# Counting masks in a routing search on TensorE: three token blocks as one 120-column stationary part, totals by one matmul over ones, and the expert's first product issued earlier

## The reference

```python
# 1: linear attention with decay, B=4, H=8, S=768, head 48
for t in range(S):
    y[:, :, t] = einsum('bhd,bhde->bhe', rt, state + u * kt * vt)
    state = w * state + kt * vt
# 2: mixture of experts, N=3072 tokens, D=384, E=8, F=1024, cap = N // E = 384
for idx in argsort(-(x @ w_gate).flatten()):       # best (token, expert) pairs first
    tok, e = idx // E, idx % E
    if assigned[tok] >= 0 or counts[e] >= cap: continue
    assigned[tok] = e; counts[e] += 1
for e in range(E):
    out[assigned == e] = relu(x[assigned == e] @ w1[e]) @ w2[e]
# 3: bilinear layer, width 1536
return ((out @ w_a) * (out @ w_b)) @ w_out
```

## Time and profile before

| | us |
|---|---|
| median of 3 runs | 968.44 (968.01 to 969.39) |
| the profiled execution | 963.17 |
| its span, first to last instruction | 961.4 |
| TensorE busy in it | 899.6 (94%) |
| VectorE, GpSimd, ScalarE busy | 517.8, 474.4, 219.2 |

### The profile page before, as it was taken

One profiled execution on the slowest core, in us unless ns is written; L12 is line 12 of the kernel. 1 busy time (PEld: TensorE's weight loads), 2 busy tenths in 40 slices (PEclk: granted clock), 3 DMA queues, 4 the chain that ended last, 5 costly groups with the idle time before them and its releaser, 6 DMA issues.

```text
span 961.4 us, 17913 instructions
## 1 busy us (share of the span) xinstructions
PE 899.6 (94%) x6581; PEld 864.7 (90%) x6581; DVE 517.8 (54%) x1238; ACT 219.2 (23%) x454; POOL 474.4 (49%) x491
## 2 busy tenths in 40 slices
PE   5999999626999999999999999999999999999995
PEld 5999999515999999999999999899999999999995
DVE  7777777575656555555545565556455622442221
ACT  0212120002123221322222223122312322222221
POOL 5988897126316731781277037604750673277001
PEclk9999999856999999999999999999999999999998
DMA  5785754003001200210021012101210221022000
GB/s 104 210 220 117 197 122 107 19 33 107 18 19 65 66 33 33 74 49 25 33 82 57 8 45 86 49 0 55 76 49 0 72 73 36 34 83 66 1 1 25
DMA packets 92782, 61.19 MB, mean 64 GB/s; under 512 B 78800, under 2 KB 83536, under 8 KB 92752
## 3 DMA queue, kind: packets, MB, share of 16 engines
q0 software_dynamic: 11008, 34.61, 11.4%
q1 hardware_dynamic: 77872, 21.45, 9.7%
q10 hardware_dynamic: 3872, 4.72, 1.4%
HBM read 51.33 MB, written 9.44 MB: 63 GB/s over the span
## 4 chain that ended last, share of the span: by engine, by line
PE 74%; issue 9%; DVE 7%; POOL 5%; DMA 3%; ACT 2%; POOLq 0%; DVEq 0%; ACTq 0%
PE bank L1060 28%; PE bank L1103 11%; PE bank L1134 9%; PE bank L972 5%; PE bank L990 4%; PE bank L1017 3%; DMA wst<-in_moe_w,rows_i 3%; PE bank L948 2%; POOL w L478 2%; POOL wst L461 2%; PE bank L996 2%; PE bank L1116 2%; PE bank L982 2%; PE bank L962 2%; DVE ga L805 1%
## 5 line engine op out<-in xcount | busy, mean ns | idle before, releaser
L1060 PE MATMUL bank<-act,w_all 128*128 128x384 f32 x1584 | 295.5, 337 | 0.0
L1060 PEld LDWEIGHTS bank<-act,w_all 128*128 128x128 f32 x1584 | 275.0, 188 | 0.5
L461 POOL DMA_INDIRECT wst<-in_moe_w,rows_i x48 | 52.1, 1086 | 272.9 <-DVE rows_i L681 216.8
L1134 PE MATMUL bank<-w_all,gs 128*128 128x384 f32 x864 | 168.2, 339 | 0.6 <-DVE gs L808 0.5
L1134 PEld LDWEIGHTS bank<-w_all,gs 128*128 128x128 f32 x864 | 149.4, 188 | 2.0 <-DVE gs L808 1.5
L478 POOL TENSOR_TENSOR w<-wst,w 128x384 fp32r<-128x384 f32 (+1 forms) x106 | 129.5, 1222 | 43.7 <-ACT w L900 38.0
L805 DVE TENSOR_TENSOR ga<-ga,bank 128x384 f32<-128x384 f32 x96 | 53.2, 554 | 149.7 <-PE bank L1060 112.6
L1103 PE MATMUL bank<-hs,w 128*128 128x384 f32 x576 | 113.4, 341 | 1.0 <-DVE hs L784 1.0
L1103 PEld LDWEIGHTS bank<-hs,w 128*128 128x128 f32 x576 | 99.8, 188 | 2.5 <-issue 1.7
L1060 PE MATMUL bank<-act,w 128*128 128x384 f32 x504 | 99.9, 342 | 0.0
L465 POOL DMA_INDIRECT wst<-in_moe_w,rows_i x64 | 67.7, 1058 | 50.3 <-POOL w L478 35.8
(11 more groups left out here) (165 smaller groups left out, 1144.3 us busy)
## 6 DMA issues: line engine op xcount, KB each, us to landing
rt<-in_r SPq DMA_DIRECT2D x24, 192.0 KB, 2.7
kt<-in_k SPq DMA_DIRECT2D x24, 192.0 KB, 3.9
vt<-in_v SPq DMA_DIRECT2D x24, 192.0 KB, 4.2
x_rows<-xs ACTq DMA_DIRECT2D x24, 192.0 KB, 3.4
raw<-in_moe_w_a SPq DMA_DIRECT2D x3, 768.0 KB, 5.9
raw<-in_moe_w_b SPq DMA_DIRECT2D x3, 768.0 KB, 6.9
raw<-in_moe_w_out SPq DMA_DIRECT2D x3, 768.0 KB, 7.0
wst<-in_moe_w,rows_i POOLq DMA_INDIRECT x112
```

The source lines that it names most:

```text
L461: pool.indirect_dma_start(wst[:, k % STAGES, :], None, w1_rows, bass.IndirectOffsetOnAxis(ap=rows_i[:, k:k + 1], axis=0)).then_inc(wst_lan ...
L1060: last = pe.matmul(dst, wt(a), mv(b), start=(n == 0 and (a, b) == (0, 0)), stop=(n == len(pairs) - 1 and (a, b) == (1, 0)))
L1134: last = pe.matmul(acc[t][:, 0:D], gs2[:, c % 2, a, t * P:t * P + P], wo2[:, b, c, :], start=(c == 0 and (a, b) == (0, 0)), stop=(c == FFC ...
```

## The change

- The search has 40 candidates instead of 41 (steps of 41 x 41, 41 and 1 as before, counted from 1), and 16-bit values are fp16 instead of bf16.
- **Counts of experts 1 to 6** (route_count): the mask is the stationary part. Three blocks of 128 tokens lie side by side, 3 x 40 = 120 columns, and their want blocks, 3 x 8 = 24 columns, move. Eight matmuls give 120 x 24 sums, of which own_tile keeps the three blocks of 8 on the diagonal (own), which are added up (sums, 120 x 8) and laid out so that partition p holds its sums at its candidate's place and zero elsewhere (spread, 120 x 320). One matmul by ones over 120 partitions and 320 columns (route_total) gives every partition all 40 x 8 counts; VectorE takes the best expert of each candidate (best), hit, hits, base.
- **The first search** (first_count, route_first): 24 matmuls with one mask block stationary (40 columns) and its want block moving (8 columns); best over 8 experts, flag, one matmul by ones with one moving column (first_hits), base.
- The places of both move; the final matmul goes from ("b", 3) to ("a", 4), and the third group of numbers from ("a", 8) to ("b", 8).
- **Expert work**: first_up(i + 1) is issued before the last product of expert i, and the high and low parts of hidden block 0 are made at the end of expert i, ahead of route_keys on VectorE and of the output copies on ScalarE.
- GpSimd's preamble makes own_tile and own_cand, seven instructions.
- The first search steps on a semaphore of its own (hole_step).

```diff
-    ROUNDS, CAND = 3, 41
-    STEPS = [CAND ** (ROUNDS - 1 - q) for q in range(ROUNDS)]
-    assert CAND ** ROUNDS >= 1 << 16 and CAP * E == N and CAP % P == 0 and H * DH == D
+    ROUNDS, CAND = 3, 40
+    STEPS = [(CAND + 1) ** (ROUNDS - 1 - q) for q in range(ROUNDS)]
+    PACK = P // CAND
+    GROUPS = NT // PACK
+    PC = PACK * CAND
+    assert NT % (2 * PACK) == 0
+    assert (CAND + 1) ** ROUNDS >= 1 << 16 and CAP * E == N and CAP % P == 0 and H * DH == D
     BIG = 1e38
...
+        flag = sb("flag", [CAND, 1], F16)
+        own_tile = sb("own_tile", [PC, PACK, E])
+        own_cand = sb("own_cand", [PC, CAND])
...
+        spread = onehot_mem[0:PC, 0:CAND * E].rearrange("p (c e) -> p c e", e=E)
...
         route = bank[7]
-        pCnt = route[0:E, 0:CAND]
-        pAny = route[:, 64:64 + CAND]
+        pCnt = route[0:PC, 0:PACK * E].rearrange("p (s e) -> p s e", e=E)
+        pTotal = route[:, 32:32 + CAND * E].rearrange("p (c e) -> p c e", e=E)
+        pFirst = route[0:CAND, 0:E]
+        pHits = route[:, 32:33]
         pFin = route[:, 128:128 + NT * E].rearrange("p (j e) -> p j e", e=E)
...
-        COUNT_AT = [("down", 0), ("down", 2), ("down", 4), ("down", 6), ("a", 1), ("b", 2)]
-        ANY_AT = [("up", 2), ("up", 4), ("up", 6), ("down", 7), ("b", 1), ("last", 1)]
-        FINAL_AT, BEFORE_AT = ("b", 3), ("a", 5)
-        NUMBERS_AT = [("last", 5), ("b", 7), ("a", 8)]
+        COUNT_AT = [("down", 1), ("down", 3), ("down", 5), ("down", 7), ("last", 0), ("last", 1)]
+        TOTAL_AT = [("up", 3), ("up", 5), ("up", 7), ("a", 1), ("a", 2), ("b", 3)]
+        FINAL_AT, BEFORE_AT = ("a", 4), ("a", 5)
+        NUMBERS_AT = [("last", 5), ("b", 7), ("b", 8)]
...
+            sp.sem_inc(dve_step, CHAIN)
...
-            step(pool.iota(cand_no[:, :], [[1, CAND]], base=0, channel_multiplier=0, **iota))
+            step(pool.iota(cand_no[:, :], [[1, CAND]], base=1, channel_multiplier=0, **iota))
...
                 link(m, dve.tensor_copy(key_hi[:, :], code[:, 0, :]))
-            def route_flags(m, q):
+            def route_sums(m, q):
                 dve.wait_ge(cnt_done, m * (2 * ROUNDS) + (q + 1))
-                dve.tensor_scalar(flag[:, :], pCnt, float(CAP), None, ALU.is_ge).then_inc(flag_ready, 1)
+                link(m, dve.tensor_tensor(own[:, :, :], pCnt, own_tile[:, :, :], ALU.mult))
+                link(m, dve.tensor_reduce(sums[:, :], own[:, :, :].rearrange("p s e -> p e s"), AX, ALU.add))
+                dve.tensor_tensor(spread, sums[:, :].rearrange("p (o e) -> p o e", o=1).to_broadcast([PC, CAND, E]),
+                                  own_cand[:, :].rearrange("p (c o) -> p c o", o=1).to_broadcast([PC, CAND, E]),
+                                  ALU.mult).then_inc(spread_ready, 1)
             def route_narrow(m, q):
                 step = STEPS[q % ROUNDS]
-                dve.wait_ge(any_done, m * (2 * ROUNDS) + (q + 1))
-                link(m, dve.tensor_scalar(hit[:, :], pAny, 0.5, float(step), ALU.is_ge, ALU.mult))
+                dve.wait_ge(total_done, (m - 1) * (2 * ROUNDS) + (q + 1))
+                link(m, dve.tensor_reduce(best[:, :], pTotal, AX, ALU.max))
+                link(m, dve.tensor_scalar(hit[:, :], best[:, :], float(CAP), float(step), ALU.is_ge, ALU.mult))
                 link(m, dve.tensor_reduce(hits[:, :], hit[:, :], AX, ALU.add))
-                link(m, dve.tensor_scalar(base[:, :], hits[:, :], -float(step), base[:, 0:1], ALU.add, ALU.add))
+                link(m, dve.tensor_tensor(base[:, :], hits[:, :], base[:, :], ALU.add))
+                route_next(m, q)
+            def route_first(q):
+                dve.wait_ge(cnt_done, q + 1)
+                link(0, dve.tensor_reduce(best[0:CAND, 0:1], pFirst, AX, ALU.max))
+                dve.tensor_scalar(flag[:, :], best[0:CAND, 0:1], float(CAP), None, ALU.is_ge).then_inc(flag_ready, 1)
+                dve.wait_ge(hits_done, q + 1)
+                link(0, dve.scalar_tensor_tensor(base[:, :], pHits, float(STEPS[q % ROUNDS]), base[:, :],
+                                                 ALU.mult, ALU.add))
+                route_next(0, q)
+            def route_next(m, q):
                 if q == ROUNDS - 1:
...
+            def lower_hidden(i, f):
+                dve.wait_ge(hs_hi, i * FC + (f + 1))
+                dve.scalar_tensor_tensor(hs2[:, f % 2, 1, :], ring[f % 2][:, 0:CAP], 0.0,
+                                         hs2[:, f % 2, 0, :].bitcast(F32), ALU.max, ALU.subtract
+                                         ).then_inc(hs_lo, 1)
             def expert(i, more, search):
...
-                    if search and f == 0:
+                for f in range(1, FC):
+                    lower_hidden(i, f)
+                    if search and f == 1:
                         candidates(i + 1, key_hi[:, :], STEPS[0])
-                    if search and f % 2 == 1:
-                        route_flags(i + 1, f // 2)
-                    if search and f % 2 == 0 and f >= 2:
+                    if search and f % 2 == 0:
+                        route_sums(i + 1, f // 2 - 1)
+                    if search and f % 2 == 1 and f >= 3:
                         route_narrow(i + 1, f // 2 - 1)
...
                 if search:
-                    route_narrow(i + 1, 3)
+                    route_sums(i + 1, 3)
                 for c in range(FFC):
-                    if search and c == 2:
-                        route_flags(i + 1, 5)
                     dve.wait_ge(as_ready, i * FFC + (c + 1))
...
                                       ALU.subtract).then_inc(gs_lo, 1)
-                    if search and c == 0:
-                        route_flags(i + 1, 4)
                     if search and c in (1, 2):
+                        route_sums(i + 1, 3 + c)
+                    if search and c in (0, 1, 2):
                         route_narrow(i + 1, 3 + c)
...
                         route_ids(i + 1)
+                assert not search or made[0] == CHAIN
                 if more:
                     lower_tokens(i + 1)
+                    lower_hidden(i + 1, 0)
             route_keys(0)
...
             for q in range(2 * ROUNDS):
-                route_flags(0, q)
-                route_narrow(0, q)
+                route_first(q)
             route_expert(0)
...
+            lower_hidden(0, 0)
...
                 act.activation(hi, src, ACT.Copy).then_inc(w_hi, 1)
+            def upper_hidden(i, f):
+                act.wait_ge(h_done, i * FC + (f + 1))
+                act.activation(hs2[:, f % 2, 0, :], ring[f % 2][:, 0:CAP], ACT.Relu).then_inc(hs_hi, 1)
             def expert(i, more):
-                for f in range(FC):
-                    act.wait_ge(h_done, i * FC + (f + 1))
-                    act.activation(hs2[:, f % 2, 0, :], ring[f % 2][:, 0:CAP], ACT.Relu).then_inc(hs_hi, 1)
+                for f in range(1, FC):
+                    upper_hidden(i, f)
                 for c in range(DC):
...
                     upper_tokens(i + 1)
+                    upper_hidden(i + 1, 0)
                 act.wait_ge(o_flushed, 1 + i)
...
             def route_count(m, q):
+                for g in range(GROUPS):
+                    if g % (GROUPS // 2) == 0:
+                        pe.wait_ge(mask_ready, m * (4 * ROUNDS) + (2 * q + 1 + 2 * g // GROUPS))
+                    last = pe.matmul(route[0:PC, 0:PACK * E], mask_mem[:, g * PC:g * PC + PC],
+                                     want[:, g * PACK:g * PACK + PACK, :].rearrange("p s e -> p (s e)"),
+                                     start=(g == 0), stop=(g == GROUPS - 1))
+                last.then_inc(cnt_done, 1)
+            def route_total(m, q):
+                pe.wait_ge(spread_ready, (m - 1) * (2 * ROUNDS) + (q + 1))
+                pe.matmul(route[:, 32:32 + CAND * E], ones[0:PC, :], onehot_mem[0:PC, 0:CAND * E],
+                          start=True, stop=True).then_inc(total_done, 1)
+            def first_count(q):
                 for j in range(NT):
                     if j % (NT // 2) == 0:
-                        pe.wait_ge(mask_ready, m * (4 * ROUNDS) + (2 * q + 1 + 2 * j // NT))
-                    last = pe.matmul(pCnt, want[:, j, :], mask[:, j, :], start=(j == 0), stop=(j == NT - 1))
+                        pe.wait_ge(mask_ready, 2 * q + 1 + 2 * j // NT)
+                    last = pe.matmul(pFirst, mask_mem[:, j * CAND:j * CAND + CAND], want[:, j, :],
+                                     start=(j == 0), stop=(j == NT - 1))
                 last.then_inc(cnt_done, 1)
-            def route_any(m, q):
-                pe.wait_ge(flag_ready, m * (2 * ROUNDS) + (q + 1))
-                pe.matmul(pAny, ones[0:E, :], flag[:, :], start=True, stop=True).then_inc(any_done, 1)
+            def first_hits(q):
+                pe.wait_ge(flag_ready, q + 1)
+                pe.matmul(pHits, ones[0:CAND, :], flag[:, :], start=True, stop=True).then_inc(hits_done, 1)
             def route_final(m):
...
```

(27 more changed lines are left out.)

74 lines of the change are left out of this document (48 added, 26 removed).

## The result

The changed kernel is **slower**, by 0.8%: 975.44 us median of five runs (974.31 to 977.70) beside 968.44 (967.60 to 969.96) of the kernel before, a ratio of 1.0076 with a 95% interval of 1.0057 to 1.0095. The forecast was 952.8, its range 945 to 965. The profiled execution took 977.70 (span 975.9).

What follows compares the result with a forecast made beforehand. TensorE was taken to bound the expert stage, a dependency chain the hole between attention and experts. Savings 16.9 + 3.5 + 0.55 + 2.1 less 7.4 of waits, 15.7 us, gave 947.5 profiled, 952.8 us median; range 945 to 965.

Steps and rivals of the forecast that it cites:

- The rest of VectorE's work hides; that cover is what I have to test: Expert stage: VectorE's remaining work costs TensorE nothing, beyond 3.5 us lost in seven places to the third slot-number group.
- rival 3: Count and total matmuls: 120 columns or rows break TensorE's pipeline at both edges; slower, 976.4 us, chance 0.06.
- Sum: Whole kernel: 16.9 - 7.4 + 3.5 + 0.55 + 2.1 = 15.7 us saved.
- The count and the totals: Search rounds on TensorE: count 0.55 us, total 0.25; a round 0.80 instead of 1.27, 16.9 us saved.
- rivals 1 and 2: 120-column count loads: first, as quick as 128, 947.9 us, chance 0.2; second, full price, 963.8 us, chance 0.17.
- Fourth count: Fourth search round: TensorE waits 0.88 us for VectorE's masks in each of six experts.
- fifth total: Fifth search round's total matmul: TensorE waits 0.35 us for VectorE's spread in each of six experts.
- Third group of slot numbers: Placed one group of products later, TensorE's waits for it all go: 3.5 us saved.
- First hidden block early: first_up ahead of the last product: nothing gained in most experts, 0.55 us in the first.
- The hole: First search between attention and experts, with nothing covering it: six times 0.35, 2.1 us saved.
- Rival 4: VectorE waits in every round, its queue delays meeting spread: 14.4 us given back, 967.2 us, chance 0.05.

Runs made afterwards that it cites:

- a_slot224: The changed kernel with VectorE's loop kept, its first instruction placed at slot 224 of a block of 256 in the instruction stream: 952.21 us.
- a_unroll: The changed kernel with VectorE's expert loop written out six times, other engines' loops kept: 947.13 us.
- a_hint: The changed kernel with VectorE's loop kept and the jump back announced at the top of its body: 954.86 us.
- b_pad42: The kernel before with 42 empty instructions added to VectorE's loop body, 276 in all: 980.23 us.
- b_pad_slot128: The kernel before with 42 empty instructions in VectorE's loop body and the loop's first instruction at slot 128 of a block of 256: 969.65 us.
- experiment 5: Trace comparison, no run of its own: GpSimd's gathers of weight rows beginning 0.04 us or more after VectorE's 1024-element comparison take 1.61 to 2.01 us, others 0.96 to 1.14.
- b_unroll: The kernel before with VectorE's expert loop written out, nothing else: 968.39 us.

## Why the prediction was wrong

**What failed is the step "The rest of VectorE's work hides; that cover is what I have to test".** I tested it operation by operation, with durations, and never asked what VectorE's added instructions do to its code; the sum put that at nothing. They push the loop's body into a third block: five pauses, 23.2 us (a_slot224 against the changed kernel), shown by taking them away (a_unroll, a_hint, a_slot224) and by putting them into the kernel before (b_pad42, undone by b_pad_slot128). Writing the loop out gives 28.3; the other 5.1 go, as far as the traces show, with the gathers of experiment 5. None of the four rivals had this mechanism; rival 3, the one on the slower side, gave 976.4, close to what was measured, but by luck: a count costs 0.42 us, not 1.07. A rule of the Trainium skill spoke against the change, and I weighed another one.

Without the pauses the steps stand like this:

- **Sum.** 15.7 us taken from the profiled 963.17 gives 947.5; a_unroll took 947.13. That agreement is partly luck: between medians the change is worth 21.3 us without the pauses, not 15.7. I added 5.3 us back because the median of before lies that far above its profiled execution. But an ordinary execution of before is slower in ways that the change removes. In b_unroll's trace an expert takes 93.0 us, not 91.7. Its down(0) comes 0.5 us later behind its up(1) (2.10 after its start) than in the earlier trace rows's expert at 415.67, where nothing waited (417.23 to 418.80, 1.57), and the third group of slot numbers waits 0.78 us instead of 0.41:

```profile
420.20 1.72 PE L1060 MATMUL bank<-act,w 128*128 128x384 f32 x9
422.30 1.84 PE L1103 MATMUL bank<-hs,w 128*128 128x384 f32 x9 [0.37 <-DVE hs L784]
```

- **The count and the totals**, 0.55 and 0.25: measured 0.42 and the rest of 0.72, about 0.30. A round saves 0.55 us instead of 0.47, 19.8 us instead of 16.9. The 0.05 for a load was right (0.052), and with it the choice against rivals 1 and 2. The late start that I put at 0.05 ahead of each count is not there. On rival 2: 16-bit loads of 120 columns do cost more than those of 128, 0.052 us against 0.028. The Trainium skill, "TensorE: Matmul & The Clock Gate", section "Weight-path perf modes", has the fast load for exactly 128 weights only, and the runs agree. The 0.1 us for 120, an estimate from the formula in its section on LDWEIGHTS, is twice what they show.
- **Fourth count 0.88, fifth total 0.35.** Right in place and size: between the end of the products ahead (350.90 + 18 x 0.173 + 0.13 = 354.15, the 0.13 being how late they start behind the total) and the next product at 355.51 lie 1.36 us, 0.94 more than a count takes; the total comes 2.07 us after the product that follows its count (364.00 to 366.07) instead of 1.67, so 0.40 late. That moving them wins back 7.3 us, as the 7.4 said, needed one more move on VectorE.
- **Third group of slot numbers.** Gone but for 0.3 us in two places. Right.
- **First hidden block early.** I had 0.55 us; 5.5 were measured, 4.2 of them in the first expert. The place was right, the size was not: I counted the wait and left out the products at half speed behind it, although shows up(1) at 2.83 us for 1.72. I also didn't see that keys and masks start late there.
- **The hole.** In the changed kernel the first key of the hole starts at 184.68 and the first expert at 228.11, 43.4 us later; in the kernel before at 182.82 and 228.91, 46.1 us. That gains 2.7 us, where I had 2.1.
- **Rival 4** did not come: the totals wait 1.4 us in all.

## What to carry to other kernels

Before adding instructions to a looped engine, count its loop body, register instructions included: keep it within two fetch blocks, give it a slot, or write it out, and look at the instruction packets of the page before and after. A wait of TensorE of two to three us costs more than its length here: price the slow products behind it too. Where weights are 16 bit, try a stationary part filled to 128 columns even if the last eight are rubbish.
